# The last two pairs of token tiles: widths 480 and 480 in place of 512 and 448

## What is computed

```python
def _attn_ref(q, k, v, tau):                       # q, k, v: (1, 6016, 256)
    qn = q / (np.linalg.norm(q, axis=1, keepdims=True) + 1e-06)
    kn = k / (np.linalg.norm(k, axis=1, keepdims=True) + 1e-06)
    s = kn.transpose(0, 2, 1) @ qn / tau           # 256 x 256
    s = s - s.max(-1, keepdims=True)
    a = np.exp(s)
    a /= a.sum(-1, keepdims=True) + 1e-09
    return (v @ a).astype(np.float32)

def _moe_ref(x, w_in, w_out):                      # 256 -> 2048 -> 256
    h = x @ w_in
    g = h * (1.0 / (1.0 + np.exp(-1.702 * h)))
    return (g @ w_out).astype(np.float32)

def _moe2_ref(x, w_in, w_out):                     # 256 -> 2048 -> 256
    h = x @ w_in
    g = np.where(h > 0.0, h, np.exp(np.minimum(h, 0.0)) - 1.0)
    return (g @ w_out).astype(np.float32)

# result: _moe2_ref(_moe_ref(_attn_ref(q, k, v, tau)))
```

## Time and profile before

| what | value |
|---|---|
| executions | 1044.15 us median of 3 (1043.72 to 1048.12) |
| the profiled execution: its own time | 1043.21 us |
| its span, first to last instruction | 1041.5 us |
| TensorE busy | 1026.1 us (99%) |
| VectorE busy | 762.5 us (73%) |
| ScalarE busy | 765.7 us (74%) |
| granted TensorE clock, mean | 0.998 of full speed |
| transfers | 46.26 MB, mean 44 GB/s |

### The profile page before, as it was taken

The page is one execution under the profiler, slowest core; times in us unless marked ns, Lnnn a source line. Parts: engine busy times, 40 slices in busy tenths (PEclk is TensorE's granted clock), DMA queues, the critical chain, the costliest instruction groups (busy, mean ns, idle before and its releaser), DMA issues.

```text
span 1041.5 us, 14053 instructions
## 1 busy us (share of the span) xinstructions
PE 1026.1 (99%) x4638; PEld 861.2 (83%) x4638; DVE 762.5 (73%) x1239; ACT 765.7 (74%) x1372; POOL 24.3 (2%) x25
## 2 busy tenths in 40 slices
PE   9999999999999999999999999999999999999996
PEld 8878888888888888889987887887887888788895
DVE  6897766565656665556778988888888887887875
ACT  7896665575665666566778888788788788788884
POOL 4400000000000000000000000000000000000000
PEclk9999999999999999999999999999999999999999
DMA  9912012012003002003122002101101201110112
GB/s 352 297 37 52 1 41 42 1 40 42 1 19 61 1 1 59 1 1 122 41 82 76 0 1 61 21 1 53 29 1 41 36 5 36 21 21 1 21 21 36
DMA packets 106936, 46.26 MB, mean 44 GB/s; under 512 B 90864, under 2 KB 97776, under 8 KB 106224
## 3 DMA queue, kind: packets, MB, share of 16 engines
q1 hardware_dynamic: 106864, 45.36, 16.2%
HBM read 33.03 MB, written 12.32 MB: 44 GB/s over the span
## 4 chain that ended last, share of the span: by engine, by line
PE 85%; ACT 5%; DVE 5%; issue 3%; DMA 1%; SPq 1%; DVEq 0%; ACTq 0%
PE bank L1016 28%; PE bank L1018 28%; PE bank L1017 28%; DVE gated L837 1%; DMA qk<-in_k_dram 1%; ACT xo L640 1%; ACT act_out L574 1%; SPq L298 1%; ACT g_hi L592 1%; DVE g_lo L850 1%; DVE sums L727 0%; ACT stage L433 0%; ACT blk_hi L498 0%; DVE blk_lo L804 0%; ACT u L534 0%
## 5 line engine op out<-in xcount | busy, mean ns | idle before, releaser
L1016 PE MATMUL bank<-g_hi,w_dn_hi 128*128 128x512 f32 (+1 forms) x768 | 296.2, 386 | 2.0 <-DVE g_lo L850 1.9
L850 DVE TENSOR_TENSOR g_lo<-gated,g_hi 128x512 fp32r<-128x512 f32 (+1 forms) x384 | 260.0, 677 | 49.4 <-ACT g_hi L592 43.4
L1017 PE MATMUL bank<-g_lo,w_dn_hi 128*128 128x512 f32 (+1 forms) x768 | 295.8, 385 | 0.0
L1018 PE MATMUL bank<-g_hi,w_dn_lo 128*128 128x512 f32 (+1 forms) x768 | 295.8, 385 | 0.0
L1016 PE MATMUL bank<-blk_hi,w_up_hi 128*128 128x512 f32 (+1 forms) x672 | 260.7, 388 | 3.5 <-DVE gated L837 2.4
L1018 PE MATMUL bank<-blk_hi,w_up_lo 128*128 128x512 f32 (+1 forms) x672 | 258.9, 385 | 0.0
L1017 PE MATMUL bank<-blk_lo,w_up_hi 128*128 128x512 f32 (+1 forms) x672 | 258.9, 385 | 0.0
L592 ACT CAST g_hi<-gated 128x512 fp32r<-128x512 f32 (+1 forms) x288 | 175.6, 610 | 21.2 <-DVE gated L837 21.2
L1016 PEld LDWEIGHTS bank<-g_hi,w_dn_hi 128*128 128x128 f32 x768 | 144.2, 188 | 30.2 <-DVE g_lo L850 3.2
L1018 PEld LDWEIGHTS bank<-g_hi,w_dn_lo 128*128 128x128 f32 x768 | 144.2, 188 | 27.1
L1017 PEld LDWEIGHTS bank<-g_lo,w_dn_hi 128*128 128x128 f32 x768 | 144.2, 188 | 26.9
(11 more groups left out here) (118 smaller groups left out, 761.0 us busy)
## 6 DMA issues: line engine op xcount, KB each, us to landing
qk<-in_q_dram SPq DMA_DIRECT2D x14, 384.0 KB, 10.0
qk<-in_k_dram SPq DMA_DIRECT2D x14, 384.0 KB, 10.6
x_scratch<-xo SPq DMA_DIRECT2D x10, 512.0 KB, 3.1
raw<-x_scratch SPq DMA_DIRECT2D x5, 1024.0 KB, 5.1
out_dram<-blocks SPq DMA_DIRECT2D x40, 128.0 KB, 2.7
blocks<-in_v_dram SPq DMA_DIRECT2D x36, 128.0 KB, 3.3
stage<-in_moe_w_in_dram SPq DMA_DIRECT2D x8, 512.0 KB, 7.5
stage<-in_moe_w_out_dram SPq DMA_DIRECT2D x8, 512.0 KB, 4.7
```

What stands on the lines that cost most here:

```text
L850: nc.vector.tensor_tensor(g[1][:, x, 0:w], gated[:, n % 2, 0:w], g[0][:, x, 0:w].bitcast(F32), ALU.subtract).then_inc(c_glo, 1)
L1016: nc.tensor.matmul(out_ps, w_hi, x_hi, start=start, stop=False, skip_group_check=goes_on)
L1017: nc.tensor.matmul(out_ps, w_hi, x_lo, start=False, stop=False, skip_group_check=goes_on)
L1018: return nc.tensor.matmul(out_ps, w_lo, x_hi, start=False, stop=stop, skip_group_check=goes_on)
```

## The change

A list of widths replaces the rule for the last pair: pairs 0 to 3 keep tiles of 512, and pairs 4 and 5 both have tiles of (6016 - 4 x 1024) / 4 = 480. `width` and `row_of` read the list. Everything that asks for the width of pair 4 or 5 follows: matmuls, copies, nonlinearities, transposes and transfers. The number of pairs, units and instructions and their order stay as they are, and so do all waits.

```diff
     assert (C, KC * P, NM * P, STEPS * P) == (2 * P, C, F, N)
-    assert sum(G_STEPS) == STEPS and (N - (NP - 1) * 2 * T) % (2 * B) == 0
+
+    WIDTHS = [T] * (NP - 2) + [(N - (NP - 2) * 2 * T) // 4] * 2
+    assert sum(G_STEPS) == STEPS and 2 * sum(WIDTHS) == N and all(w % B == 0 for w in WIDTHS)
 
     q_t = q[0].rearrange("(p s) c -> p s c", p=P)
     k_t = k[0].rearrange("(p s) c -> p s c", p=P)
 
     def width(p):
-        return T if p < NP - 1 else (N - (NP - 1) * 2 * T) // 2
+        return WIDTHS[p]
 
     def row_of(p, tile):
-        return p * 2 * T + tile * width(p)
+        return 2 * sum(WIDTHS[:p]) + tile * width(p)
```

## The result

The changed kernel takes 1047.05 us (median of 22 runs, 1044.68 to 1049.68), the kernel before 1044.16 us (median of 22, 1042.91 to 1048.12). The ratio is 1.0023, with a 95% interval of 1.0016 to 1.0031: 1.7 to 3.2 us slower, a small difference but a real one. Its profiled execution took 1047.17 us with a span of 1045.5, so 4.0 us more than that of before.

The account below looks back on a forecast made before the run. TensorE, busy 99% of the span, was taken as the bound: matmul count times pitch. Pitch 0, segment 5 -0.6, layer change 0, transfers 0, tail +0.2 sum to -0.4 us: 1044.15 to 1043.7 us, range 1040.8 to 1047.5.

Parts of the forecast that it names:

- the pitch at 480: Start-to-start distance of 480-wide matmuls, 720 pairs: 214.65 ns halfway between 512 and 448, change 0, range -1.8 to +1.8 us.
- Rows 4 to 7: Profile rows of matmul starts: 226.7 ns at 512, 202.6 and 206.8 at 448, 117.5 at 256 columns.
- My outer end: Highest reading of the 480 pitch: 20.1 ns on top of the columns, 220.1 ns, +7.8 us.
- The sign of being wrong: Prediction counts as wrong if 480's pitch lies outside 211 to 218.5 ns or the layer change moves over 2 us.
- No floor from the weight load at 448: The 188 ns weight load doesn't hold up the 448 pitch, since 256 columns with as many loads take 117.5 ns.
- Segment 5: Where second-layer weights are prepared: wider tiles give TensorE cover, 0.6 us of 1.0 excess gained, bounds 0 and 1.0.
- Change of layer: Segment 6, 4.4 us of waiting: taken as unchanged, 0, bounds -0.3 and +0.3 us.
- Transfers, segment changes of layer 2, segment 4: Pair 4's scratch transfer in pieces has 27 us of cover; layer-2 segment changes and segment 4's cover unchanged: each 0.
- Tail: From 1027.64 us, beside its matmuls: longer dependent instructions, transposes and stores, +0.2 us, bounds 0 and +0.4.
- The high pitch of 220.1 ns: First rival: 480 settles in a state like 448's higher one in all four segments, 1051.5 us, chance 0.05.
- whole 64s: Rival: TensorE rounds up to multiples of 64 columns, 480 costs 226.7 ns, +17.4 us, 1061 us, chance 0.02.
- The faster one (210.8 ns): Rival: 480 pitch as 256's part on top gives, -5.5 us, and segment 5's whole 1.0 us gained; about 1037.9 us, chance 0.04.

Follow-up runs that it names:

- The streams: Only TensorE's matmul triples, everything else of the kernel left out, at many widths, then bfloat16, other columns and after other widths; float32r 216.7 ns at 480, 202.7 at 448.
- 480 then 448: Changed kernel with pair 4 480 wide and pair 5 448, last 64 tokens left out; time not comparable, segment 5 took 74.06 us.
- the sweep: Changed kernel with pairs 512, 480, 448, 416, 384 and 352 wide, last 832 tokens left out; time not comparable, segment 5 (352) took 62.4 us.
- the six bare streams after a gap: TensorE alone, 60 matmuls each after a short wait for VectorE, three streams at 448 and three at 480; they settled at 202.7 and 216.7 ns.
- 448 early: Changed kernel with pair 1 448 wide and all others 512; 1043.08 us, ratio 0.9988 to the kernel before; repeated 1043.32 us, 0.9991.
- 480 early: Changed kernel with pairs 1 and 2 480 wide and all others 512; 1046.51 us, ratio 1.0018 to the kernel before.
- the exchange: Kernel before with its last two pairs exchanged, pair 4 448 wide and pair 5 512; 1043.76 us, ratio 0.9998.

## Why the prediction was wrong, point by point

- **The median, 1043.7 forecast, 1047.05 measured.** Still inside the range (1040.8 to 1047.5), and within 0.5% of before as forecast, but I had the sign wrong: -0.4 forecast, +1.7 to +3.2 measured. That the range held it is no merit of the working: the terms alone ended at 1046.7 us, and the rest was added for the spread of the first three runs. And 0.5% is not the least that the runs can tell: 22 of each resolved 0.23%.
- **The step that failed is the pitch at 480.** I took the straight line between the rows of 512 and 448, change 0, with +1.8 us as the upper bound, on the grounds that 480 lies between two steady widths. It has 16.7 ns on top, more than 512 and the usual state of 448, and the term is +2.9 us. The streams show why this interpolation missed it: 480 lies on a line that runs from 464 to 504 columns, and both neighbours that I used lie below that line. Rows 4 to 7 had given a warning, three widths with four values on top; that was a reason not to trust the mean of two neighbours. My outer end (220.1 ns, +7.8 us) covers the real value, and I gave all between 215.9 and that end too little weight.
- **The sign of being wrong** was set too wide: a pitch outside 211 to 218.5 ns. The measured 216.7 lies inside, and yet by the prediction's own sum the change turns from a gain to a loss at 214.65 + 0.4 us / 1440 = 214.9 ns.
- **No floor from the weight load at 448:** right, and now borne out. 64 columns of weights leave the pitch at 480 and 448 as it is within 0.5 ns, and 256 columns have 119.8 ns. The load isn't free at every width, though: at 256 the narrower weights take 6 ns off.
- **The rule of the Trainium skill** (TensorE: Matmul & The Clock Gate, Back-to-back issue gap) of width / 2.4 ns plus about 2.5, which the page gives as the gap of an isolated matmul: here it holds for bfloat16 streams with a weight load each (about 2.5 ns on top at 480 and 448) and does not hold for float32r, where the streams have 11.8 to 20 ns on top.
- **Segment 5:** -0.6 forecast with 1.0 as the bound, -0.9 measured. The mechanism was right and the size within its bounds: 0.6 us of it were waits, and 0.3 the higher pitch of the earlier trace rows. 480 then 448 brings the waits back (0.8 us), and 352 loses 4.1 us.
- **Change of layer:** 0 forecast, and 4.4 us over the sum of pitches before and after. That is partly luck: a fall of the clock that the prediction didn't have costs about 0.3 us, and it cancels what the wider tiles ahead give back, below.
- **Transfers, segment changes of layer 2, segment 4:** 0 forecast; -0.1 us in all. The 21.7 us given as free in segment 4 is a slip: 81.6 - 49.9 = 31.7 us. It only makes the case for 0 stronger.
- **Tail:** +0.2 us forecast beside the matmuls, +0.05 measured.
- **The rivals.** The high pitch of 220.1 ns didn't come; the second state that it rested on is real at 448, but none was found at 480; nor did whole 64s, since 480 differs from 512. The faster one (210.8 ns) didn't come either. The real case, p = 216.7, lay between the forecast's 215.9 and the first rival's 220.1, where no case had been named.

## What to carry to other kernels

When TensorE never waits, the time is a count times a pitch, and the pitch of a width must be measured at that width. Two good neighbours didn't give it here. A bare stream did, to 0.1 ns of what the real kernel has; but it should also be run after other widths, since 448 and 496 showed two pitches each. With a fixed total of columns compare the sums of what lies on top (here 13.3 + 16.0 ns for 512 and 448 against 2 x 16.7 for 480 twice), not the evenness of the split. If one tile must be narrow, look for a place where the other engines have slack: 448-wide tiles in the segment where they prepare weights lost 1.0 us, and 0.1 in layer 1 as pair 1 or as pair 4 (73.61 us each time, against a sum of 73.5).

## What the runs showed of the hardware that I had not expected

- Float32r matmuls with a new weight load each, from 256 to 512 columns, have 12 to 20 ns on top of the columns, up and down with the width; at 448 and 496 there are two pitches (202.7 or 206.7, 220.0 or 223.3 ns), which go with what ran before. Where the columns start in their tile matters too at 480 (216.7 against 217.8 ns). Bfloat16 has 2.5 ns at 480 and 448. What makes the curve and the states stays open: no run here looks inside it.
- In the kernel before, the state of 206.8 ns began at the gap of the earlier trace rows and ended at the next gap, and cost 0.3 us. A gap can end it in other kernels too: in segment 8 of the sweep and in segment 11 of 480 then 448, the 448-wide matmuls have 206.7 ns up to the gap in the second unit, and 202.7 behind it. That a gap also begins the state was seen once only; the six bare streams after a gap and the gaps in segment 5 of 480 then 448 didn't do it.
- After the change of layer the clock can fall. The changed kernel and the one before, three microseconds each after the gap:

```profile
551.00:554.00 3.00, 2.83 (x7) 2.37 (x8) 1.92 (x4) 2.31 (x5) 0.00 (x0) 0.55 0.00 0
```

```profile
550.00:553.00 3.00, 3.00 (x15) 2.50 (x14) 1.58 (x3) 2.94 (x7) 0.00 (x0) 1.00 0.08 31
```

In the changed kernel the granted clock is 0.55 on average, so mostly at the 1.2 GHz level, and the window touches 7 matmuls in place of 15. The 512-wide ones in it start 427 ns apart while it lasts. What TensorE did before it fell (changed kernel, timeline):

```profile
549.67 0.49 PE L1018 MATMUL bank<-g_hi,w_dn_hi 128*128 128x480 f32 x1 [1.15 <-DVE g_lo L852]
551.17 0.65 PE L1018 MATMUL bank<-blk_hi,w_up_hi 128*128 128x512 f32 x1 [0.57 <-DVE blk_lo L806]
```

Before the change it waited 1.25 us at the same place and kept the 2.4 GHz level. The kernel before has waits of its own a few microseconds later (one of 1.0 us, at 556.94), which the changed one has not; so both have 4.4 us over the sum of pitches in segment 6, by different ways. The width ahead doesn't decide it. With 512 ahead the clock stays up in one kernel and falls in another (segment 6, first of 448 early, then of 480 early):

```profile
537.58:623.05 85.47, 82.92 (x361) 67.12 (x360) 70.51 (x117) 71.95 (x129) 0.00 (x0) 1.00 0.11 36
```

```profile
539.82:625.59 85.77, 84.18 (x362) 68.36 (x360) 70.81 (x117) 72.15 (x129) 0.00 (x0) 0.98 0.11 37
```

At the same widths the fall costs 0.3 us, and the exchange (85.78 us, clock fallen) and the second profile of 448 early (85.48, clock up) show the same. With the clock up, segment 6 is 4.4 us over its sum of pitches behind tiles of 448 and 3.9 behind tiles of 512, so wider tiles ahead do give cover. What makes the clock fall in one and not in the other stays open.
